# Interleaving the chunks of two sequences, and making the first two chunks' block products on TensorE, in a fused linear-attention and two-MLP kernel

## The reference

```python
for t in range(S):                      # state is (B, H, D, D)
    cur = einsum('bhd,bhe->bhde', u * k[t], v[t])
    y[t] = einsum('bhd,bhde->bhe', r[t], state + cur)
    state = w * state + einsum('bhd,bhe->bhde', k[t], v[t])
x = y as (B*S, H*D)
x = (silu(x @ w_gate) * (x @ w_val)) @ w_out                     # first MLP
x = x / sqrt(mean(x*x) + 1e-6) * rms_g                           # then the second MLP
out = (silu(x @ w_gate2) * (x @ w_val2)) @ w_out2
```

## Time and profile before

| | |
|---|---|
| median of 3 runs | 997.33 us (996.99 to 998.04) |
| profiled execution, its own time | 996.6 us |
| its span, first to last instruction | 994.7 us |
| TensorE busy | 959.1 us, 96% of the span |
| VectorE, GpSimd, ScalarE busy | 704.7, 565.5, 401.8 us |
| moved by DMA | 136.06 MB |

### The profile page before, as it was taken

How to read it: one execution, slowest core, us unless ns; L and a number is a source line. 1 busy time by engine, 2 the same in 40 slices (tenths; PEclk the granted TensorE clock), 3 DMA queues, 4 the chain that set the end, 5 groups by cost and what they waited for, 6 DMA issues and landing times.

```text
span 994.7 us, 23699 instructions
## 1 busy us (share of the span) xinstructions
PE 959.1 (96%) x9324; PEld 794.8 (80%) x9324; DVE 704.7 (71%) x1123; ACT 401.8 (40%) x839; POOL 565.5 (57%) x446
## 2 busy tenths in 40 slices
PE   4898999999999999999999999999999999999998
PEld 4898997888888888888877777787888777878876
DVE  7888677576857756675429968788677899567760
ACT  3463334334333433433432454434633436344423
POOL 8898986556666666466233325678526787211134
PEclk9999999999999999999999999999999999999999
DMA  6663443535434343543142156443064441254201
GB/s 256 217 216 112 141 148 115 176 116 176 176 130 149 130 149 108 179 151 110 64 154 85 42 182 222 159 149 116 33 220 152 147 159 54 102 174 159 80 0 64
DMA packets 50348, 136.06 MB, mean 137 GB/s; under 512 B 6656, under 2 KB 9664, under 8 KB 50240
## 3 DMA queue, kind: packets, MB, share of 16 engines
q1 hardware_dynamic: 50240, 134.56, 38.5%
HBM read 108.29 MB, written 25.17 MB: 134 GB/s over the span
## 4 chain that ended last, share of the span: by engine, by line
PE 73%; POOL 9%; DVE 8%; issue 7%; DMA 2%; ACT 1%; POOLq 0%; SPq 0%; DVEq 0%; ACTq 0%
PE ps_down L810 7%; PE ps_down L812 6%; PE ps_down L811 6%; PE ps_val L810 6%; PE ps_val L811 5%; PE ps_val L812 5%; PE ps_gate L810 5%; PE ps_gate L812 5%; PE ps_gate L811 5%; PE ps_level L903 4%; PE ps_level L1056 2%; PE ps_level L1058 2%; PE ps_level L1057 2%; PE ps_val L956 1%; PE ps_val L1056 1%
## 5 line engine op out<-in xcount | busy, mean ns | idle before, releaser
L1827 POOL TENSOR_TENSOR h_lo<-h_raw,h_hi 128x512 fp32r<-128x512 f32 (+1 forms) x84 | 114.8, 1367 | 203.1 <-ACT h_hi L1162 194.3
L810 PE MATMUL ps_down<-h_hi,down_hi 128*128 128x512 f32 (+1 forms) x360 | 134.9, 375 | 0.9 <-DVE room_c L1671 0.9
L812 PE MATMUL ps_down<-h_lo,down_hi 128*128 128x512 f32 (+1 forms) x360 | 132.6, 368 | 0.0
L811 PE MATMUL ps_down<-h_hi,down_lo 128*128 128x512 f32 (+1 forms) x360 | 132.6, 368 | 0.0
L1162 ACT ACTIVATE h_hi<-h_raw 128x512 fp32r<-128x512 f32 (+1 forms) x84 | 47.9, 571 | 153.5 <-DVE h_raw L1428 153.4
L1428 DVE TENSOR_TENSOR h_raw<-h_raw,ps_val 128x512 f32<-128x512 f32 (+1 forms) x84 | 51.1, 608 | 82.9 <-PE ps_val L812 75.0
L810 PE MATMUL ps_gate<-x_hi,up_weights 128*128 128x512 f32 (+1 forms) x252 | 93.9, 373 | 2.2 <-ACT h_raw L1156 1.3
L810 PE MATMUL ps_val<-x_hi,up_weights 128*128 128x512 f32 (+1 forms) x249 | 90.9, 365 | 5.2 <-DVE h_raw L1428 3.3
L812 PE MATMUL ps_gate<-x_lo,up_weights 128*128 128x512 f32 (+1 forms) x252 | 91.0, 361 | 0.3 <-issue 0.3
L1870 POOL TENSOR_TENSOR pair_prod<-chunk_in,w_block 128x768 f32<-128x768 f32 x47 | 91.3, 1943 | 0.0
L811 PE MATMUL ps_gate<-x_hi,up_weights 128*128 128x512 f32 (+1 forms) x252 | 90.9, 361 | 0.0
(11 more groups left out here) (293 smaller groups left out, 2456.5 us busy)
## 6 DMA issues: line engine op xcount, KB each, us to landing
ring<-sums_dram SPq DMA_DIRECT2D x72, 640.0 KB, 4.8
r_block<-in_r_blk_dram SPq DMA_DIRECT2D x24, 768.0 KB, 4.9
chunk_in<-in_a_t_dram SPq DMA_DIRECT2D x24, 512.0 KB, 3.6
chunk_in<-in_a_n_dram SPq DMA_DIRECT2D x24, 384.0 KB, 4.4
sums_dram<-sum_lo SPq DMA_DIRECT2D x24, 320.0 KB, 3.0
staging<-in_weights_dram SPq DMA_DIRECT2D x18, 384.0 KB, 4.0
raw<-in_blocks_dram SPq DMA_DIRECT2D x8, 576.0 KB, 5.4
sums_dram<-sum_hi SPq DMA_DIRECT2D x12, 320.0 KB, 2.4
```

The costliest lines, as they stand in the source:

```text
L810: nc.tensor.matmul(dst, w_hi, x_h, start=first, stop=False)
L811: nc.tensor.matmul(dst, w_lo, x_h, start=False, stop=False)
L812: return nc.tensor.matmul(dst, w_hi, x_l, start=False, stop=last)
L1827: nc.gpsimd.tensor_tensor(h_lo[:, f % 3, 0:WIDTH[t]], h_raw[:, f % 2, 0:WIDTH[t]], h_hi[:, f % 3, 0:WIDTH[t]].bitcast(F32), ALU.subtract). ...
```

## The change

**Chunks in turn.** A table `CHUNK_AT` says which chunk stands at place g: places 0 to 11 take the chunks of sequences 0 and 1 in turn, places 12 to 23 those of sequences 2 and 3. The host lays out inputs and puts the results back by it. A chunk's state comes from place g-2, and `state` has three places in turn. Both of the first two chunks open a sequence, so neither has a state before it; `for_carried` makes only half for those.

**Blocks of four of the first two chunks.** For places 0 and 1 (`BY_LEVELS`) `weigh_k`, `multiply_pairs`, `sum_pairs` and `take_block` go, and the two `r_block` transfers. In their place ScalarE makes `k_fine` and `r_fine` (`scale_fine`: ten instructions a chunk), VectorE and GpSimd make `r_two` and `k_two` (`scale_two`), TensorE makes all pairs of a block of two and the level of two (`fine`: 32 calls), and VectorE puts both in through masks (`take_fine`). The third level of these two chunks is taken by VectorE too, no more by ScalarE.

**The opening in order.** The two chunks' transfers by channel stand first, then masks, then the chunks by step, two pieces, the table of weights, and two more pieces. `sums` of chunk 1 is cut in two by halves (`second_sums`). `first_result` does one half of the result after the other, behind two matmuls by zeros that open the first half's bank. Piece 1 goes from GpSimd to VectorE, piece 2 to GpSimd, piece 4 to VectorE. The levels of chunk 2 stand behind slot 3 (before: 1).

**Matmuls of ones.** `keep_up` issues fp32 matmuls of ones, 128x128 by 128 columns, whose result nobody reads: 11 ahead of the first level, one behind the second chunk's result, one behind its `fill`.

```diff
-EARLIEST = (1, 15, 27)
+EARLIEST = (3, 15, 27)
+FIRST_SCALE = (1, 1, 2, 2)
+UP_FIRST, UP_RESULT, UP_FILLED = 11, 1, 1
-WEIGHED_HERE = (1,)
-POOL_PIECES = (1, 4, 7, 10, 13, 16)
+CHUNK_AT = [(g // (2 * CPB) * 2 + g % 2) * CPB + g % (2 * CPB) // 2 for g in range(NCH)]
+BY_LEVELS = 2
+WEIGHED_HERE = ()
+POOL_PIECES = (2, 7, 10, 13, 16)
 # SyncE, the opening
             sp.dma_start(w_pow[:, 0, :], w_t).then_inc(w_in, 16)
+            sp.dma_start(u_in[:, :], u_t).then_inc(u_loaded, 16)
             load_steps_last(0)
+            load_steps_last(1)
+            (level_mask, fine_mask, turns)
             load_steps_first(0)
+            load_steps_first(1)
+            for j in range(2):
+                load_piece(j)
             (w_blk, w_last)
-            (level_mask, block_mask, turns)
-            load_steps_last(1)
-            load_r_block(0)
-            load_steps_first(1)
-            for j in range(STAGING):
+            for j in range(2, STAGING):
                 load_piece(j)
+            load_r_block(2)
+            (block_mask)
             (gain)
-            load_r_block(1)
             load_chunk(2)
-            load_r_block(2)
             load_piece(STAGING)
 # TensorE
+            def fine(g):
+                pe.wait_ge(fine_scaled, g + 1)
+                reach(pe, fine_in, 2 * g)
+                (16 matmuls k_fine by r_fine, 64 columns, into pairs_out)
+                pe.wait_ge(r_two_done, g + 1)
+                pe.wait_ge(k_two_done, g + 1)
+                (16 matmuls k_two by r_two, 32 columns, into twos_out; fine_done)
+            def first_result(g):
+                pe.wait_ge(fine_in, 2 * BY_LEVELS)
+                pe.wait_ge(high_in, g + 1)
+                pe.wait_ge(pow_moved, 2)
+                (2 matmuls zeros by r_fine, 256 columns)
+                pe.wait_ge(r_state_done, g + 1)
+                pe.wait_ge(mid_done, g + 1)
+                (from_state of slot 0: 4; from_tokens of half 0: 8; from_state of slot 1: 4; from_tokens of half 1: 8; y_done)
+            def keep_up(n, place):
+                for _ in range(n):
+                    nc.tensor.matmul(place, pow_up[:, 0, 0:1].broadcast_to([P, P]), pow_up[:, 0, 0:1].broadcast_to([P, P]),
+                                     start=True, stop=True, skip_group_check=True)
+            pe.wait_ge(one_in, 1)
+            keep_up(UP_FIRST, ps_gate[:, 0:P])
             for l in range(LOW):
                 level(0, l)
+            fine(0)
             turn_powers()
             level(0, LOW)
             for l in range(LOW):
                 level(1, l)
+            fine(1)
             sums(0)
+            second_sums(0)
             level(1, LOW)
-            for g in range(SIZES[0]):
-                if g:
-                    sums(g)
-                carried(g, 0)
-                carried(g, 1)
-                own(g)
-                fill(g)
-            pe.wait_ge(pow_nat_done, 1)
+            first_result(0)
+            second_sums(1)
+            fill(0)
+            first_result(1)
+            keep_up(UP_RESULT, ps_down[:, 0, 0:P])
+            fill(1)
+            keep_up(UP_FILLED, ps_down[:, 0, 0:P])
             begin_val()
 # ScalarE
+            scale_fine(0)
+            scale_fine(1)
             (turn of the powers)
-            take_third(0)
-            take_high(0)
             (pow_nat)
+            take_high(0)
             split_piece(0)
-            take_third(1)
+            split_piece(1)
             take_high(1)
-            split_piece(1)
+            split_piece(2)
             copy_last(0)
             copy_first(0)
-            split_piece(2)
             copy_last(1)
             copy_first(1)
 # VectorE, behind the start of the ladder of powers
+                if l == 0:
+                    scale_two(0)
+                elif l <= LEVELS:
                     scale_r(0, l - 1)
+            scale_two(1)
             for l in range(LOW):
                 scale_r(1, l)
-            (multiply_pairs, sum_pairs, take_block of chunks 0 and 1)
+            take_low(0, 0 to 2); take_fine(0); scale_r(1, LOW); take_low(1, 0 to 2); take_fine(1)
+            dve.wait_ge(fine_in, 2 * BY_LEVELS)
+            (half_near and pow_near copied into their bank; pow_moved)
+            sum_mid(0); sum_mid(1); split_piece(0); sum_end(0); sum_end(1); split_piece(1)
+            first_lo(0); first_lo(1); split_piece(3)
 # VectorE, tile 0: scale_r(2, l) behind slots 1, 1, 2, 2, and split_piece(4) at slot 3
 # GpSimd: weigh_k of chunks 0 and 1 gone; scale_two(0) behind scale_k(0, 2); for_sums(0), scale_k(1, 3), for_sums(1),
 # for_carried(0) and (1), then the table w_block, split_piece(2), scale_k(2, l), weigh_k(2, half)
```

415 lines of the change are left out of this document (270 added, 145 removed).

## The result

The changed kernel takes 1001.15 us (median of 6 runs, 999.62 to 1002.76), the kernel before 997.22 beside it (996.42 to 998.04). The ratio is 1.0038, 95% interval 1.0025 to 1.0051: slower by 3.8 us, where the prediction had 6.3 us less than before. The profiled execution took 1000.04 with a span of 997.9, 3.2 more than the span of before.

The account below looks back on a forecast made before the run. TensorE, busy for 96% of the span, was taken as the bound, so the change could gain only in the first 40 us: -4.5 - 2.1 + 0.3 = -6.3 us, from 996.6 to 990.3 profiled, 991.0 as median, range 987 to 998.

Parts of the forecast that it names:

- Parts 1 and 2: Opening: some 13 us of VectorE's work go with the blocks of four; the first level starts at 7.1 instead of 5.90.
- Part 3: Chunk 1's levels: TensorE stops for instructions after 218 matmuls, near 13.7 us, and goes on at 17.4.
- second rival: Clock lost on the way: it falls in the opening, `begin_val` near 31.5 to 32.5, time about 994.5 us; 22%.
- first of its rivals: Full speed in the opening, no stop for instructions: `begin_val` at about 26.3, time 987.9 us; 12%.
- Part 4: From the stop's end to `begin_val`, all at full speed: `begin_val` at 29.4 instead of 33.94, 4.5 us less.
- A wait that returns: Chunk 1's levels: the kernel before's stop for instructions, 15.73 to 18.47, was expected again near 13.7 us.
- third rival: Half speed throughout the opening: `begin_val` at 35.7, 1.8 later, nothing saved behind it, time 999.1 us; 15%.
- Part 5: First groups behind `begin_val`: at full speed they take 3.1 us instead of 5.25, 2.1 less.
- Part 6: Tile 0 loses 0.3 us, bounds 0 and 1.7; a later chunk changes by 0, between -0.3 and 0.3.

Follow-up runs that it names:

- early_1: The changed kernel with the levels of chunk 2 behind slot 1 again, not slot 3: 1001.45 us, ratio 1.0029.
- scale_early: The changed kernel with the four `scale_r` of chunk 2 moved from tile 0's slots into the opening: 1002.08 us, ratio 1.0040.
- pool_early: The changed kernel with GpSimd's `for_sums(2)` and `for_carried(2)` moved out of tile 0's slots into the opening: 998.56 us, ratio 1.0014.
- pool_early_mixed: pool_early with the carried calls in the order of the kernel before: 997.64 us, ratio 1.0000.
- carried_mixed: The changed kernel with the carried calls taking the two slots in turn, as in the kernel before: 999.68 us, ratio 1.0020.
- combined: The changed kernel with 13 more ones before chunk 1's levels, chunk 2's `scale_r` in the opening and the old carried order: 999.65 us, ratio 1.0022.
- no_ones: The changed kernel without any matmul of ones (13 calls taken out): 999.27 us, ratio 1.0016.
- offset_160: pool_early_mixed with 40 matmuls of 32 columns ahead of the first level in place of all its ones: 1008.90 us, ratio 1.0106.
- offset_224: pool_early_mixed with 56 matmuls of 32 columns ahead of the first level in place of all its ones: 1014.91 us, ratio 1.0175.
- small_29: The changed kernel with 29 matmuls of 32 columns ahead of the first level and no ones: 1002.11 us, ratio 1.0044.
- before_small_11: The kernel before with 11 matmuls of 32 columns ahead of the first level: 1002.54 us, ratio 1.0046.
- offset_20: pool_early_mixed with 5 matmuls of 32 columns ahead of the first level in place of all its ones: 996.34 us, ratio 0.9989.
- before_ones: The kernel before with 11 matmuls of ones ahead of the first level: 1002.19 us, ratio 1.0047.
- ones_kept: The changed kernel with 35 more calls of ones between the steps of the opening: 1001.33 us, ratio 1.0056.

## Why the prediction was wrong

**Parts 1 and 2** held. The blocks of four are gone from VectorE's and GpSimd's path, `fine(0)` took 1.5 us from 9.53, and the first level began at 6.90 (7.1 said). The ones are hidden as said: 5.06 us, 0.92 of waiting left.

**Part 3** held for the place (218 said, 220 counted in the profile), and for the mechanism, now with more behind it. The end was mis-sized: I took 17.4, between the same length and the same moment, and it was neither. It was 14.71, 1.5 us behind a packet that came 3.9 us earlier than in the kernel before. "A wait that returns" was misread too: in the kernel before the stop cost its path some 0.2 us of the 2.75, since VectorE's products lay beside it; with these gone it stands on the path in full. *By the Trainium skill (Runtime: NRT & Kernel Launch, Instruction fetch mechanics) crossing a block is mostly hidden. The runs agree with "mostly": of the changed kernel's 76 packets four are seen as a stop of over 0.3 us. Those seen in all runs cost 0.3 to 3.1 us each.* The prediction says there that by this rule the sum would be that of the second rival; a chain with no stop is the first of its rivals.

**Part 4 is the step that failed first.** It took full speed for the chain from 17.4 us on. The clock did rise, at 10.3, and fell at 13.7, before the chain that Part 4 sums had begun: the second rival, the clock lost on the way, in its time that of the third. The prediction named two things that could let it fall, the stop or the small matmuls behind the ones. The fall at 13.7 lies 0.2 us into the stop, but six profiles have the same matmuls up to there, and the clock is up from 10.3 to 13.7 in the changed kernel, from 3.9 to 7.3 and 10.7 to 14.1 in early_1, 4.1 to 7.5 in scale_early, 6.0 to 9.4 in pool_early, 3.8 to 7.2 and 10.6 to 14.0 in pool_early_mixed, and 5.9 to 9.3 and 12.7 to 16.1 in carried_mixed. In five of the six it falls by 9.4, well before any stop for instructions. So the stop isn't needed for the fall, and by combined and no_ones it doesn't suffice for it; what decides it in this opening stays open. What all six show is that the clock was at 1.2 GHz from 16.1 us at the latest until `begin_val`.

Full speed would not have been enough either, and that is the second thing that Part 4 left out: it counts no stop behind the first. combined had the clock up until 24.8, stopped for instructions for 5.3 us in three places, and had `begin_val` at 33.91.

The size of the third rival, the half-speed chain, was right: it has 35.7 from a stop that ends at 17.4, which is 33.0 from one that ends at 14.71, and the second stop of 0.87, which the prediction didn't count, makes 33.9. `begin_val` came at 33.98. That it fits to 0.1 us is luck in part: up to `first_result(0)` (22.51) the trace has 1.1 us more than the sum besides the stop, and behind it 1.0 less.

Without stops that chain is 24.3 us from the first level (offset_160, offset_224), where the kernel before had 28.04. The stop of 2.75 can't be taken off the 28.04, for VectorE's products lay beside it. So what the blocks of four as levels bring is up to 3.7 us at this clock. The changed kernel's 27.08 gives back 2.8 of it, 2.04 in the two stops and most of the rest in the 1.00 of waiting for `take_low` at 11.81, and the start that is 1.0 later takes what is left.

**Part 5** fell with it: 3.62 us from `begin_val` to the rise of the clock at 37.6. (In the kernel before the clock's first record is at 38.3, not at the 39.2 that the prediction read from the starts.) The saving is there where the clock is (small_29), and was gone again by 95 us.

**Part 6 was mis-sized twice.** I took 0.3 us for tile 0, looking at VectorE; the loss was 0.65 of lag, and by pool_early 1.5 us could be had there. The prediction named GpSimd as 99% busy and "through 5.5 us behind `begin_val`", and didn't ask what comes when it is through earlier (1.6 us behind it, at 35.6): it then waits 3.44 and 3.14 us in front of work that was tied to slots, with chunk 2's own work queued behind. And I put a later chunk at 0 within 0.3; the order of the carried calls, which the change alters as well, costs 0.3 between the 37th and the 72nd silu alone, and more likely 0.5 to 1 in all.

**What was missing** is a term: stops for instructions behind the opening, +1.5 us in the profile (1.81 against 0.33). Part 3 had the mechanism in hand, counted matmuls for the first cut, and did not ask what the 146 matmuls more do to all other cuts. before_small_11 shows it on the kernel before, and offset_20 on the mended one, in the places of the stops.

The account in the profile's terms: opening +0.05, tiles 0 and 1 +0.65, stops behind 40 us +1.5, the rest +1.0, of which the carried order may be most. pool_early_mixed undoes the second and the order and is level with the kernel before (1.0000 [0.9991, 1.0009]); in its profile offset_20 has half of the third gone as well. What stays open is what lets the clock fall in the opening, why the second packet of instructions ends anywhere from 17.7 to 19.2 us in kernels whose bytes ahead in the queue are the same, with stops at 346 of 0.9 to 3.1 us, and why `r_block` lands 1.7 us later in before_ones and before_small_11.

## What to carry to other kernels

Where one engine issues hundreds of small matmuls in a row, count its instructions: added or removed ones move all later cuts, and 44 that did nothing cost the kernel before 4.6 us, in the opening and behind it. Before a gain is booked at the higher clock, ask if the instructions come fast enough for it (126 matmuls a packet here, and in the changed kernel's opening one packet in 3.5 to 4.7 us) and what keeps the clock up; here it fell even where no stop stood. Before a stop is counted as a cost, look which engine's work lies beside it: 2.75 us held VectorE up for 0.23 in one kernel, and in the other 1.17 and 0.87 stood on TensorE's own path. And when work leaves a saturated engine whose order is written by hand, move what stood behind it forward too: the gain was in a hole of 3.44 us in front of work that could have been done there.

## What the hardware showed that I had not expected

- Stops for instructions stand at fixed counts of TensorE's matmuls (220, 346, 472, ..., 4078), whatever lies there; the same count in up to ten kernels.
- Ones of 128 by 32 cost as much as ones of 128 by 128: 0.215 us a recorded matmul at the lower clock (24.10 us for 112) against 0.23 (5.06 for 22).
- A stop's end follows the instruction queue: in 19 profiles TensorE went on 1.2 to 1.7 us behind the end of a packet, from 14.5 us as at 425.
- The clock stayed at 2.4 GHz through stops of 1.24 and 2.18 us in combined and of 1.05 in no_ones, and fell at 7.2 to 9.4 us in five profiles with no stop for instructions before.
- In offset_224 TensorE was busy for 24.07 of 24.07 us with narrow ones and for 22.89 of 24.30 with small matmuls behind them, and the clock didn't rise until 55.4, 6 us into the large ones. In ones_kept it had been up from 4.0 to 7.4 and rose again at 17.6, behind 10.2 us of ones, levels and `fine` with no gap.
- In nine of the 17 profiles the clock fell for a while somewhere between 77 and 103 us, around a chunk's stage (in before_ones from 99.1 to 102.5, and the lag of that kernel rises by 1.4 us there). Neither kernel of the comparison had it in its profile.
